# Attention, soft MoE and FFN on one core: scores in 64x64 tiles, a new order of the step, and a reordered tail

## What is computed

```python
B, H, S, D = 4, 8, 768, 48
for t in range(S):                       # 1: linear attention with decay w and bonus u
    cur = u * k[t] (outer) v[t]
    y[t] = r[t] @ (state + cur)
    state = w * state + k[t] (outer) v[t]
x = y as [3072 tokens, 384]              # 2: soft mixture, 8 experts of 4 slots
logits = x @ phi                         #    [3072, 32]
d = softmax(logits over tokens);  c = softmax(logits over slots)
slot_out[e] = relu((d.T @ x)[e] @ w1[e]) @ w2[e]
x = c @ slot_out
h = x @ w_in                             # 3: FFN, 384 -> 2048 -> 384
out = (h * sigmoid(1.702 * h)) @ w_out
```

## Time and profile before

| | us |
|---|---|
| median of 3 runs | 388.12 (387.99 to 388.98) |
| the profiled execution: its own time | 389.18 |
| its span, first to last instruction | 387.4 |
| PE busy | 376.3 (97%) |
| DVE busy | 230.4 (59%) |
| ACT busy | 186.2 (48%) |
| POOL busy | 111.8 (29%) |
| mean granted clock of PE | 0.991 |

### The profile page before, as it was taken

How to read it: one execution, slowest core, us unless ns; L and a number is a source line. 1 busy time by engine, 2 the same in 40 slices (tenths; PEclk the granted TensorE clock), 3 DMA queues, 4 the chain that set the end, 5 groups by cost and what they waited for, 6 DMA issues and landing times.

```text
span 387.4 us, 9097 instructions
## 1 busy us (share of the span) xinstructions
PE 376.3 (97%) x3228; PEld 295.5 (76%) x3228; DVE 230.4 (59%) x420; ACT 186.2 (48%) x410; POOL 111.8 (29%) x122
## 2 busy tenths in 40 slices
PE   7899999999999999989999999999999999999996
PEld 6778787877876344667888888888888888888885
DVE  6677878788774301467655565555556655655560
ACT  1235354545434441486555546554655465455552
POOL 5888798787682020264200000000000000000000
PEclk9699999999999999999999999999999999999999
DMA  7899999999999999700002001000200020002002
GB/s 233 288 313 379 395 382 400 390 364 372 393 332 414 369 376 417 272 0 2 1 0 84 0 2 71 10 0 0 81 0 0 0 81 0 0 0 81 2 0 81
DMA packets 21797, 63.76 MB, mean 165 GB/s; under 512 B 3088, under 2 KB 6816, under 8 KB 21392
## 3 DMA queue, kind: packets, MB, share of 16 engines
q1 hardware_dynamic: 20432, 62.99, 43.2%
q10 hardware_dynamic: 1344, 0.49, 0.6%
HBM read 58.75 MB, written 4.72 MB: 164 GB/s over the span
## 4 chain that ended last, share of the span: by engine, by line
PE 92%; DVE 3%; DMA 2%; issue 1%; ACT 1%; SPq 0%; POOL 0%; DVEq 0%; POOLq 0%; ACTq 0%
PE bank L587 11%; PE bank L586 11%; PE bank L585 11%; PE bank L347 7%; PE pair L386 6%; PE pair L585 6%; PE pair L587 5%; PE pair L586 5%; PE bank L572 4%; PE pair L369 4%; PE pair L377 3%; PE bank L407 3%; PE bank L534 3%; PE bank L514 2%; PE bank L398 2%; DMA vb<-v 2%
## 5 line engine op out<-in xcount | busy, mean ns | idle before, releaser
L849 DVE TENSOR_TENSOR gf<-bank,sg 128x512 f32<-128x512 f32 x72 | 49.6, 691 | 63.7 <-ACT sg L1031 63.5
L1031 ACT ACTIVATE sg<-bank 128x512 f32<-128x512 f32 x72 | 42.9, 598 | 73.2 <-PE bank L572 73.1
L585 PE MATMUL bank<-glo,whi 128*128 128x512 f32 x190 | 74.0, 389 | 0.0
L586 PE MATMUL bank<-ghi,whi 128*128 128x512 f32 x190 | 74.0, 389 | 0.0
L587 PE MATMUL bank<-ghi,wlo 128*128 128x512 f32 x190 | 73.9, 389 | 0.0
L855 DVE TENSOR_TENSOR glo<-gf,ghi 128x512 fp32r<-128x512 f32 x96 | 69.1, 720 | 0.2
L1037 ACT ACTIVATE ghi<-gf 128x512 fp32r<-128x512 f32 x96 | 60.0, 625 | 0.9 <-DVE gf L849 0.9
L919 ACT ACTIVATE yt<-pair 112x512 f32<-112x512 f32 x24 | 14.3, 597 | 58.5 <-PE pair L386 58.5
L585 PEld LDWEIGHTS bank<-glo,whi 128*128 128x128 f32 x190 | 35.7, 188 | 7.5
L586 PEld LDWEIGHTS bank<-ghi,whi 128*128 128x128 f32 x190 | 35.7, 188 | 7.4
L587 PEld LDWEIGHTS bank<-ghi,wlo 128*128 128x128 f32 x190 | 35.7, 188 | 7.4
(11 more groups left out here) (176 smaller groups left out, 526.4 us busy)
## 6 DMA issues: line engine op xcount, KB each, us to landing
ring<-w SPq DMA_DIRECT2D x24, 512.0 KB, 6.2
rkb<-rk SPq DMA_DIRECT2D x23, 512.0 KB, 5.2
krb<-kr SPq DMA_DIRECT2D x24, 384.0 KB, 5.6
ring<-w SPq DMA_DIRECT2D x4, 1536.0 KB, 14.1
ring<-w SPq DMA_DIRECT2D x8, 768.0 KB, 9.1
vb<-v SPq DMA_DIRECT2D x24, 192.0 KB, 5.6
out<-ob SPq DMA_DIRECT2D x18, 256.0 KB, 2.1
ring<-win SPq DMA_DIRECT2D x3, 1024.0 KB, 15.3
```

What stands on the lines that cost most here:

```text
L585: pe.matmul(o, w_hi, lo, start=(f == 0), stop=False)
L586: pe.matmul(o, w_hi, hi, start=False, stop=False)
L849: dve.tensor_tensor(gf[:, f % 2, :], bank[f % 4][:, :], sg[:, f % 2, :], ALU.mult).then_inc(gf_ok, 1)
L1031: act.activation(sg[:, f % 2, :], bank[f % 4][:, :], ACT.Sigmoid, scale=1.702).then_inc(sg_ok, 1)
```

## The change

Seven edits.
1. `scores`: 16 matmuls of 64 columns of weights instead of 8 of 128, in 64x64 tiles.
2. `outputs` is split in three. PE's step is now: earlier product of n-1, scores of n, outputs of n-1, state of n-1, tokens of n-2, bonus turns of n. `gather` moves behind the bonus turns. A new semaphore `vd_used` frees vd, `rs_used` now only rks.
3. DVE: in step n `scale` of n+1 stands before `mask` of n (in chunk 0 after it); the bonus sum is that of n+1. (Before, `mask` of n stood in step n+1, before `scale` of n+1.)
4. Early weights: row maximum at b = 1, exponential at b = 2 (ACT), row sums at b = 2 behind the mask and before the bonus sum of the last step, multiply on POOL at b = 3 before `bonus_values`.
5. c^T is turned in the last step, into PSUM bank 5, before the last bonus turns; its low part for 512 tokens lies in ct[:, 0].
6. ACT: `decay` before `columns`.
7. Tail: spreads 1, 2, 3, 0 all before the six matmuls (before, the last one came after them), the update of acc before lf and samef, the copy of the first spread earlier on ACT.

```diff
@@ scores @@
-                    for p0, i in HEADS:
-                        s = slice(p0, p0 + D)
-                        last = pe.matmul(SC[i][:, hp * CH:(hp + 1) * CH],
-                                         rks[s, b % 2, 1, hp, :], rks[s, b % 2, 0, hp, :], start=True, stop=True)
+                    for half in HALVES:
+                        for p0, i in HEADS:
+                            s = slice(p0, p0 + D)
+                            last = pe.matmul(SC[i][half, hp * CH:(hp + 1) * CH],
+                                             rks[s, b % 2, 1, hp, half], rks[s, b % 2, 0, hp, :], start=True, stop=True)
...
@@ PE's step @@
+                if not is_first(c, b):
+                    earlier(*prev(c, b))
                 scores(c, b)
                 if not is_first(c, b):
+                    if is_first(c):
+                        bonus_turns(*prev(c, b))
                     outputs(*prev(c, b))
                     if b == 0 or not is_last(c):
                         state(*prev(c, b))
                     if tail and b == 1:
                         turns(c - 1)
-                    if tail and b == 2:
-                        gather(c - 1, LG, 2 * c)
                     if not is_first(*prev(c, b)):
                         tokens(*prev(*prev(c, b)))
+                if is_last(c) and b == B - 1:
+                    pe.wait_ge(s_new, B * (C - 1) + 1)
+                    pe.wait_ge(c_ok, 1)
+                    turned_weights(1, 0, 4)
+                if not is_first(c) or b == B - 1:
+                    bonus_turns(c, b)
+                if tail and b == 2:
+                    gather(c - 1, LG, 2 * c)
...
@@ PE's tail @@
+            earlier(C - 1, B - 1)
             outputs(C - 1, B - 1)
             tokens(C - 1, B - 2)
-            pe.wait_ge(c_ok, 1)
-            turned_weights(1, 0, 4)
-            logits(C - 1)
-            tokens(C - 1, B - 1)
...
             spread_weights(1)
+            logits(C - 1)
+            tokens(C - 1, B - 1)
+            spread_weights(2)
...
             pe.transpose(LG[:, P:2 * P], et[:, :], idt[:, :]).then_inc(te_ps, 1)
-            spread_weights(2)
+            spread_weights(3)
             gather(C - 1, bank[4], 2 * C - 1)
+            spread_weights(0)
...
-            spread_weights(3)
...
             last.then_inc(si_ps, 1)
-            spread_weights(0)
@@ DVE's step @@
-                    mask(*prev(c, b))
-                    scale(c, b)
...
-                bonus_sum(c, b)
...
+                if is_first(c) and b:
+                    mask(c, b)
+                    scale(*following(c, b))
+                else:
+                    if more:
+                        scale(*following(c, b))
+                    mask(c, b)
+                if is_last(c) and b == 2:
+                    row_sum(*early)
+                if more:
+                    bonus_sum(*following(c, b))
...
@@ DVE's tail: moved up, before lf and samef @@
+            dve.wait_ge(p_ps, C)
+            dve.scalar_tensor_tensor(acc[:, :], acc[:, :], alpha, bank[4][:, 0:DM], ALU.mult, ALU.add)\
+               .then_inc(run_ok, 1)
@@ ACT's step @@
-                if is_last(c) and b == 3:
-                    row_exp(0, EARLY)
                 if not is_first(c, b):
-                    columns(*prev(c, b))
                     if not is_last(prev(c, b)[0]):
                         decay(*prev(c, b))
+                    columns(*prev(c, b))
...
+                if is_last(c) and b == 2:
+                    row_exp(0, EARLY)
@@ POOL @@
-                wait(pool, rs_used, n - 1)
+                wait(pool, vd_used, n - 1)
...
+                if is_last(c) and b == 3:
+                    pool.wait_ge(rsum_ok, 1)
+                    pool.tensor_tensor(*row_terms(1, 0, EARLY), ALU.mult).then_inc(c_ok, 1)
                 bonus_values(c, b)
```

More of the change, by code:

```diff
@@ L39 @@
 HEADS = ((0, 0), (64, 1))
+HALVES = (slice(0, 64), slice(64, P))
 LOWEST = -3.0e38
@@ L166, in rwkv_soft_moe_ffn @@
         CT = (1, 2, 3, 5, 3, 2)
+        TURN = (None, 5, 2)
         MB = (3, 2, 7, 3)
@@ L356, in scores, with bonus_turns @@
                     keep_warm(LG, 4)
-            def outputs(c, b):
+            def bonus_turns(c, b):
                 n = B * c + b
-                if not is_first(c):
-                    wait(pe, s_new, n - 2)
                 wait(pe, yt_ok, n)
@@ L372, in outputs, with earlier @@
                                          skip_group_check=True)
-                if not is_first(c):
+                last.then_inc(vd_used, 1)
+            def earlier(c, b):
+                n = B * c + b
+                if is_first(c):
+                    pe.sem_inc(rs_used, 1)
+                else:
+                    wait(pe, s_new, n - 2)
+                    pe.sem_inc(tiles_go, 1)
                     for a in range(2):
@@ L380, in outputs @@
                                                  start=False, stop=False, skip_group_check=True)
-                last.then_inc(rs_used, 1)
+                    last.then_inc(rs_used, 1)
+            def outputs(c, b):
+                n = B * c + b
                 wait(pe, masked, 2 * n + 2)
@@ L432, in gather, with turned_weights @@
                 last.then_inc(p_ps, 1)
+            def turned_weights(which, c0, c1):
+                for c in range(c0, c1):
+                    last = pe.transpose(bank[TURN[which]][:, (c - c0) * P:(c - c0 + 1) * P],
+                                        lnat[:, c, :, :].rearrange("p b s -> p (b s)"), idt[:, :])
+                last.then_inc(cturn_ps, 1)
             def step(c, b):
@@ L786, in step @@
                 if tail and b == 3:
                     running(c - 1)
[L788 to L791, removed]
+                if not is_first(c, b) and not is_last(prev(c, b)[0]):
+                    new_state(*prev(c, b))
+                if is_last(c) and b == 1:
                     row_max(*early)
-                if is_last(c) and b == 3:
-                    row_sum(*early)
+            scale(0, 0)
@@ L796, in _ @@
+            dve.tensor_tensor(wks[a, :, :], wk[a, :, :], pw[a, 7, :].unsqueeze(2).to_broadcast([PAIR, HP, CH]),
+                              ALU.mult).then_inc(wks_done, 1)
+            bonus_sum(0, 0)
             steps(dve, step)
-            mask(C - 1, B - 1)
             def low_weights(which, t):
                 dve.wait_ge(chi_ok, which)
-                dve.tensor_tensor(clo[:, t], bank[which][:, 0:t.stop - t.start], chi[:, t],
+                dve.tensor_tensor(ct[:, 0, t] if which == 1 else clo[:, :], bank[TURN[which]][:, 0:t.stop - t.start], chi[:, t],
@@ L975, in step, with spread_out @@
                         rows(*prev(*prev(c, b)))
+                if is_last(c) and b == 2:
+                    row_exp(0, EARLY)
             def high_weights(which, t):
                 act.wait_ge(cturn_ps, which)
-                act.activation(chi[:, t], bank[which][:, 0:t.stop - t.start], ACT.Copy).then_inc(chi_ok, 1)
+                act.activation(chi[:, t], bank[TURN[which]][:, 0:t.stop - t.start], ACT.Copy).then_inc(chi_ok, 1)
             steps(act, step)
+            act.wait_ge(dd_ok, B * C)
+            high_weights(1, slice(0, 512))
             columns(C - 1, B - 1)
             rows(C - 1, B - 2)
-            act.wait_ge(dd_ok, B * C)
-            high_weights(1, slice(0, 512))
+            def spread_out(k, b):
+                act.wait_ge(ct_ps, k + 1)
+                act.activation(ct[:, b, 0:512], bank[CT[b]][:, :], ACT.Copy).then_inc(ct_ok, 1)
+            spread_out(0, 1)
             exponentials(C - 1)
@@ L994, in _ @@
             kept_logits(C - 1)
-            for k, b in enumerate((1, 2, 3, 0)):
-                act.wait_ge(ct_ps, k + 1)
-                act.activation(ct[:, b, 0:512], bank[CT[b]][:, :], ACT.Copy).then_inc(ct_ok, 1)
+            for k, b in enumerate((2, 3, 0), 1):
+                spread_out(k, b)
             act.wait_ge(tr_ps, C)
```

56 lines of the change are left out of this document (20 added, 36 removed).

## The result

The changed kernel takes **392.21 us** (median of 4 runs, 391.68 to 395.08), the kernel before takes 388.55 beside it (387.99 to 389.06). The ratio is 1.010 [1.0068, 1.0131]: slower by 0.7 to 1.3%, outside the range of the prediction. The profiled execution took 391.68 us, span 389.9, against 389.18 and 387.4 before; the 2.5 us between these two executions are what the traces can account for.

What follows compares the result with a forecast made beforehand. PE was taken to set the loop's pace, with full DMA engines right behind. Gains of 0.45 us (attention) and 0.3 us (tail) made 0.75, likeliest 1.0 us off 388.12: 387.1 us, 386.4 to 387.7; range with rivals 384.0 to 389.5.

Steps and rivals of the forecast that it cites:

- What the PE edits are worth: Loop steps 5 to 23: fewer tile-shape changes and narrower score weights save PE 0.33 us a step, 6.3 us in all.
- Why little of it arrives: Loop: DMA engines, full at 386 GB/s, cannot give the 409 needed; PE waits, and of 6.3 us only 0.45 is kept.
- rival 1: Loop: the DMA queue has room, up to a 435 GB/s ceiling; nearly all gain arrives, 381.5 up to 386.4 us; chance 0.2.
- Rival 3: Step 23: a PE wait near 1.95 us halves the clock, costing 1.7 to 3.4 us; 389.1 to 390.8 us; chance 0.14.
- Step 23: Last attention step: vd(23) done at 118.85, earlier(23) starts at 119.5 instead of 119.95, so 0.45 us gained.
- The other late steps: Last steps: scale(23) before mask(22) puts scores(23) at 115.35, against 115.32; bonus_sum behind the row sums runs until 117.25.
- Tail: From the gather on: accumulator update and spreads moved ahead free between 0 and 0.3 + 0.3 us, taken as 0.3 us.
- Downstream: Expert products start 0.75 us earlier; PE can gain 0.9 to 1.6 us before it waits there for the win weights.

Runs made afterwards that it cites:

- e5: The changed kernel with scores back in 64x128 tiles and gather ahead of the tokens: 387.49 us, ratio 0.9963.
- e10: The changed kernel with scores in 64x128 tiles and gather ahead of the tokens, run a second time: 388.06 us, ratio 0.998.
- e9: The changed kernel run again with nothing altered, beside the kernel before: 391.72 us, ratio 1.0088.
- e4: The changed kernel with gather ahead of tokens and the early weights' row sums, multiply and c^T turn late, as before the change: 389.98 us, ratio 1.0042.
- e8: The changed kernel with gather ahead of tokens, row sums behind the last bonus sum, multiply behind vd(23), c^T turned in the tail: 390.27 us, ratio 1.0037.
- e11: The kernel before with 32 unused semaphore increments a step on PE, two behind each matmul of scores and state: 444.98 us, ratio 1.148.
- e6: The changed kernel with all pieces of w1 asked for after the last step: 409.9 us in one run.

## Why the prediction was wrong, by its steps

**What the PE edits are worth: right.** Forecast 0.33 us a step (0.27 to 0.40), found (18.65 - 17.40)/4 = 0.31. Scores in 64x64 tiles do run four at a time: the block takes 0.88 us with 32 matmuls, no more than 8 rounds of 0.11. The surcharge of some 60 cycles for each matmul, which the Trainium skill has in "TensorEngine Tiling (Array Packing)", section Instruction Overhead, would by the prediction's estimate have made 0.4 us more of it; neither this block nor the earlier block (0.58 us with 16 matmuls, as before) shows it. That the two edits can be priced change by change holds for their sum only: one edit of the two alone gives 0.06 to 0.10 us a step, not its share.

**Why little of it arrives: the step that fell first.** "No iteration gives that", of 409 GB/s. The third and fourth pass ran at 399 and 404 GB/s, in 17.52 and 17.40 us, with PE at 17.52 of 17.52. A share of 1.01 at 386 GB/s was taken for the end of what the engines can move; it was what was asked of them, at a share that also reads 1.03 at 399 and 0.98 at 359. The trace of before had a hint of it: 417 GB/s in a slice. The ceiling of 435 GB/s in "DMA: Bandwidth & Descriptors", section Where 436 GB/s comes from (the Trainium skill), rival 1's rule, agrees with the traces: 404 is the highest of a pass here. The same section says that between HBM and SBUF the HBM side, about 358 GB/s a core, binds; this core moved 399 and 404 over whole passes, and the measurement decides. So the room was there, and rival 1's mechanism was the right one for the loop. By it alone the result should have been 5 us lower; the passes 2 to 4 gave 3.09.

**The first pass: a step that is missing.** Of the edit that doubles the matmuls and weight loads of the scores, only the array's time was reckoned. That PE runs 384 matmuls and 384 weight loads more (3612 for 3228, and 395 for 332 in a pass of the loop), and that the loop's code comes in through the same full DMA engines, had no term. It measured 2.98 us of stops and 1.7 of clock in this execution. Rival 3 had the clock as a mechanism, in the wrong place: it looked for the wait in step 23 (there PE did wait, for 1.08 us, and the clock held), and the fall came in the first pass, behind a stop of 1.47 us.

**Step 23: the second step that fell.** "The row maximum and its exponential come a step sooner into time in which DVE and ACT wait for rkb: nothing, unless the exponential is later than 115.3; then it is the next thing late." The condition was the right one, and it came true: the exponential ran 10.86 us after the logits, where 115.3 would be 9.6 (it is 105.7 in that trace), and everything behind it was late. What was not looked up is who holds ACT ahead of it: a copy to a buffer that the gather, moved behind the bonus turns, still had to read. Moving the gather was reckoned as tail alone. vd(23) was to be done 13.15 us after the logits, 118.85; it was 15.1. Instead of 0.45 us gained, 1.54 lost. The other late steps (scale ahead of mask, bonus_sum behind the row sums) were in time or hidden.

**Tail: right in size, half of it elsewhere.** 0.3 us forecast, 0.43 measured. From the gather's start to the experts' first product it is 3.09 us instead of 3.29 (128.55 to 131.64, before 125.81 to 129.10), so 0.20 came where 0.3 was expected; the other 0.23 came ahead of the gather, where the prediction had nothing. **Downstream: not tested**, since the attention came later, not sooner.

In sum: forecast -0.75 us for this execution; measured +2.54, of which -3.09 and -0.43 were of the predicted kind, +3.94 the first pass and +1.54 step 23, +0.58 the start.

**A version that beats both** is the changed order without its first edit: scores in 64x128 and the gather ahead of the tokens (e5 and e10), at 0.9963 [0.9943, 0.9982] and 0.998 [0.9967, 0.9994].

## What to carry to other kernels

An edit that splits instructions into smaller ones has to be priced twice: in the array, which the windows of a block show, and in code, which costs where a stretch runs for the first time, the more so when the DMA engines are full; look for idle time put down to "issue" in the middle of a block, see whether the stops of two kernels lie behind the same number of instructions, and compare the first pass of a loop with the others. Before moving an instruction back, list the buffers that it reads: whoever refills them waits, and all that is queued behind the refill. A DMA share of 1.0 with the bytes that the program asks for is no bound by itself; look in the page for slices that move more.

## What the runs showed of the hardware that was not expected

PE stops of 0.4 to 2.55 us in the first pass over its code, with no semaphore in play, and none in later passes; each ends 1.2 to 1.6 us after a 16 KB piece of code has been moved, and its place is the same one in each kernel with the same code, the first three 123 and 122 matmuls apart. 16 DMA engines at a share of 1.04 moved 404 GB/s over 17.4 us, and 386 at 1.01 was not their limit. The granted clock went to 0.50 for 3.4 us after stops of 1.47 us (the changed kernel) and 1.75 us (e9), but stayed at 1.00 after the stop of 1.51 us in the same execution, after 1.73 us in e4 and after 2.55 us in e8: the length of a stop alone doesn't tell. In e11 it fell to 0.50 three times between 35 and 87 us with no stop above 0.3 us. In e6, where PE stood idle for 13.3 us with its weights on the way, it was at 1.2 GHz for 17.1 us:

```profile
127.00:144.60 17.60, 5.76 (x28) 1.59 (x32) 0.66 (x4) 0.35 (x1) 0.00 (x0) 0.52 1.03 415
```

And semaphore increments between matmuls are not free: 32 a step took 2.7 us, at most some 85 ns each, since the lower clock has a part in it.
